# Moving two pair turns, the block table and the totals around expert block 0

## What is computed

```python
# attention: q, k, v [2, 8, 768, 64]; window |i-j| < 16, and 24 block summaries
scores = concat(where(near, q@k.T/8, -1e9), q@k_max.T/8 + log(32))
x = softmax(scores) @ concat(v, v_mean)             # -> x [1536, 512]
# MoE: 8 experts, 512 -> 1024 -> 512
logits = normed(x) @ normed(emb).T / tau
e = argmax(logits); gate = softmax(logits)[e]
x = gate * (relu(x @ w1[e]) @ w2[e])
# dense: 512 -> 2048 -> 512
h = relu(x @ w_in);  out = (h * h) @ w_out
```

## Time and profile before

| | |
|---|---|
| median of 3 runs (lowest, highest) | 553.02 (552.63, 553.21) |
| the profiled execution, its span | 553.05, 551.3 |
| PE busy | 523.8 (95% of the span), 4442 matmuls |
| DVE busy | 269.4 (49%) |
| ACT busy | 234.9 (43%) |
| POOL busy | 89.0 (16%) |
| chain that ended last: PE, SP's queue, DVE, DMA | 84%, 5%, 4%, 4% |

### The profile page before, as it was taken

How to read it: one execution, slowest core, us unless ns; L and a number is a source line. 1 busy time by engine, 2 the same in 40 slices (tenths; PEclk the granted TensorE clock), 3 DMA queues, 4 the chain that set the end, 5 groups by cost and what they waited for, 6 DMA issues and landing times.

```text
span 551.3 us, 10956 instructions
## 1 busy us (share of the span) xinstructions
PE 523.8 (95%) x4442; PEld 473.1 (86%) x4442; DVE 269.4 (49%) x442; ACT 234.9 (43%) x413; POOL 89.0 (16%) x123
## 2 busy tenths in 40 slices
PE   7498977899999999999999999999999999999997
PEld 6387866789998989989889899899989989989995
DVE  6477877768485864757462232232223223232321
ACT  5478855655676653555531231222223123122221
POOL 5761111212543131260100000000000000000000
PEclk9789999899999999999999999999999999999999
DMA  7956678895679958768110020020001002001001
GB/s 215 257 154 176 186 182 251 251 338 176 251 260 331 312 160 275 263 229 275 64 47 1 0 77 1 1 76 0 0 21 56 0 0 76 0 0 38 2 2 38
DMA packets 62655, 69.50 MB, mean 126 GB/s; under 512 B 22512, under 2 KB 47088, under 8 KB 62232
## 3 DMA queue, kind: packets, MB, share of 16 engines
q1 hardware_dynamic: 59160, 57.36, 32.9%
q0 software_dynamic: 3456, 11.60, 6.2%
HBM read 58.88 MB, written 10.06 MB: 125 GB/s over the span
## 4 chain that ended last, share of the span: by engine, by line
PE 84%; SPq 5%; DVE 4%; DMA 4%; issue 1%; ACT 1%; POOL 0%; DVEq 0%; ACTq 0%; POOLq 0%
PE psum L917 26%; PE psum L918 25%; PE psum L919 25%; DMA k_raw<-in_k 2%; SPq L364 2%; PE psum L911 1%; PE psum L765 1%; PE psum L703 1%; DMA x_rows_sb<-x_rows,gather_tab 1%; SPq L366 1%; PE psum L1021 1%; SPq L363 1%; DVE wb_lo L1627 1%; DVE neg_max L1351 1%; PE psum L830 1%
## 5 line engine op out<-in xcount | busy, mean ns | idle before, releaser
L919 PE MATMUL psum<-x_hi,win_lo 128*128 128x256 f32 x384 | 108.7, 283 | 0.0
L918 PE MATMUL psum<-x_lo,win_hi 128*128 128x256 f32 x384 | 108.7, 283 | 0.0
L917 PE MATMUL psum<-x_hi,win_hi 128*128 128x256 f32 x384 | 108.5, 282 | 0.0
L1725 DVE TENSOR_TENSOR h_sq<-h_relu 128x512 f32<-128x512 f32 x48 | 33.2, 692 | 126.6 <-ACT h_relu L1291 126.6
L1291 ACT ACTIVATE h_relu<-psum 128x512 f32<-128x512 f32 x48 | 28.7, 597 | 127.4 <-PE psum L919 127.4
L917 PE MATMUL psum<-wb_hi,h_hi 128*128 128x512 f32 x208 | 82.4, 396 | 0.0
L919 PE MATMUL psum<-wb_hi,h_lo 128*128 128x512 f32 x208 | 81.1, 390 | 0.0
L918 PE MATMUL psum<-wb_lo,h_hi 128*128 128x512 f32 x208 | 81.1, 390 | 0.0
L918 PEld LDWEIGHTS psum<-x_lo,win_hi 128*128 128x128 f32 x384 | 73.6, 192 | 1.4
L917 PEld LDWEIGHTS psum<-x_hi,win_hi 128*128 128x128 f32 x384 | 73.6, 192 | 1.4
L919 PEld LDWEIGHTS psum<-x_hi,win_lo 128*128 128x128 f32 x384 | 73.6, 192 | 0.0
(11 more groups left out here) (211 smaller groups left out, 878.2 us busy)
## 6 DMA issues: line engine op xcount, KB each, us to landing
w_raw<-in_moe_w SPq DMA_DIRECT2D x56, 512.0 KB, 4.0
win_raw<-in_moe_w_in POOLq DMA_DIRECT2D x8, 512.0 KB, 8.1
w_raw<-in_moe_w_out SPq DMA_DIRECT2D x8, 512.0 KB, 3.6
k_raw<-in_k SPq DMA_DIRECT2D x8, 384.0 KB, 3.6
q_raw<-in_q SPq DMA_DIRECT2D x8, 384.0 KB, 5.5
v_blk<-in_v SPq DMA_DIRECT2D x3, 1024.0 KB, 8.0
v_win<-in_v SPq DMA_DIRECT2D x16, 192.0 KB, 3.9
x_rows<-x_all SPq DMA_DIRECT2D x8, 384.0 KB, 5.4
```

Source lines behind the costliest of these rows:

```text
L917: pe.matmul(o, l_hi, r_hi, start=start, stop=False)
L918: pe.matmul(o, l_hi, r_lo, start=False, stop=False)
L919: return pe.matmul(o, l_lo, r_hi, start=False, stop=stop)
L1725: dve.tensor_tensor(h_sq[c % 2][:, :], h_relu[c % 2][:, :], h_relu[c % 2][:, :], ALU.mult)\
```

## The change

Routing of batch 0, in the attention's last pairs:

- `choose` is split: `read_logits` (L1487) stays in place, `row_max(3,0,0)` and `move_prob(2,1,0)` come next, then the rest of `choose(0)`.
- PE's `totals` moves behind `values(2,1,0)` and `turn_pair(4)`, from the free end of bank 5 to bank 7; it waits for DVE's copy of the last q and k out of that bank, and DVE's `move_totals` moves behind `move_pair(4)`. `fill(3,1,2)`, the next writer of bank 7, waits for `totals_moved`; before, `turn_pair(4)` did.
- `lay_blocks` is split: `lay_starts` (L1522 to L1533) stays, and the table of experts moves behind `make_hots` and `scale_out(3,0,0)`. `row_max(3,1,1)` moves behind `list_tokens`.
- `hot_tok` of batch 0 goes from DVE to POOL, ahead of the first gather in POOL's program; PE's `slots` waits for it (`toks_made`).

Turning of pairs 5 and 6: out of the attention, to behind piece 0 of block 0's up product. Pair 7 goes from behind piece 0 to behind piece 1, the logits of batch 1 from piece 1 to 2, their turning from piece 2 to 3 and into bank 5. DVE's `choose(1)` moves behind the whole up product, `totals(1)` from step (0,0) of the down product to (0,3), `ranks(1)` from (0,3) to (1,0). PE's wait for `logits_read` moves from ahead of `turn_rows(1)` to step (0,6).

Loads of block 0: before, four pieces were issued ahead of the store of x of pair 6 and the wait for the first rows; now two are.

```diff
 # SP, load_expert
-                    if first and c == PIECES:
+                    if first and c == PIECES // 2:
                         store_x(PAIRS - 2)
                         sp.wait_ge(gathered, 32)
 # POOL, ahead of gather(0)
+            pool.wait_ge(hot_hi_made, 1)
+            pool.tensor_tensor(hot_tok[:, :, :], hot_hi[:, :, :],
+                               token1[:, 0:TILES].unsqueeze(2).broadcast_to([P, TILES, HB]), ALU.mult)\
+                .then_inc(toks_made, 1)
+            pool.wait_ge(toks_made, 1)
 # PE
+            values(2, 1, 0)
+            turn_pair(4)
             pe.wait_ge(consts_made, 2)
-            pe.wait_ge(prob_moved[0], 2 * 5 + 1)
-            pe.wait_ge(prob_moved[1], 2 * 5 + 1)
-            totals(0, 5, at=GT * P)
-            values(2, 1, 0)
-            pe.wait_ge(totals_moved, 1)
-            turn_pair(4)
+            pe.wait_ge(qk_moved_dve, PAIRS)
+            totals(0, 7)
...
+            pe.wait_ge(totals_moved, 1)
             fill(3, 1, 2)
...
-            turn_pair(5)
             scores(3, 1, 1)
-            wait_turned(6)
             turn_probs(3, 0, 1)
+            pe.wait_ge(toks_made, 1)
             slots(0, 7)
...
-            turn_pair(6)
-            wait_turned(7)
             turn_probs(3, 1, 1)
 # PE, weigh_second
                 if c == 0:
...
+                    turn_pair(PAIRS - 3, bank=6)
+                    turn_pair(PAIRS - 2, bank=4)
+                elif c == 1:
+                    wait_turned(PAIRS - 1)
                     turn_pair(PAIRS - 1, bank=6)
-                elif c == 1:
+                elif c == 2:
                     wait_turned(PAIRS)
                     logits(6)
-                elif c == 2:
-                    turn_logits(1, 7)
+                else:
+                    turn_logits(1, 5)
 # PE, count_second
-                if (t, f) == (0, 0):
+                if (t, f) == (0, 3):
                     totals(1, 0)
-                elif (t, f) == (0, 3):
+                elif (t, f) == (0, FC - 2):
+                    pe.wait_ge(logits_read, 2)
+                elif (t, f) == (1, 0):
                     ranks(1, 1)
 # ACT and DVE, block 0
             for c in range(PIECES):
-                if c == 3:
-                    choose(1, 7)
                 experts_up(0, c)
                 if c == 0:
+                    move_pair(PAIRS - 3, bank=6)
+                    move_pair(PAIRS - 2)
+                elif c == 1:
                     move_pair(PAIRS - 1, bank=6)
-                elif c == 1:
+                elif c == 2:
                     move_logits(1, 6)
+            read_logits(1, 5)
+            choose(1)
```

DVE's program for the last pairs, cut:

```diff
             move_logits(0, 4)
+            read_logits(0, 5)
+            row_max(3, 0, 0)
+            move_prob(2, 1, 0)
             dve.wait_ge(consts_made, 2)
-            choose(0, 5)
-            move_prob(2, 1, 0)
-            row_max(3, 0, 0)
+            choose(0)
             move_kq(3, 1)
-            move_totals(0, 5, at=GT * P)
             scale_out(2, 1, 0)
             move_pair(4)
+            move_totals(0, 7)
...
-            lay_blocks(0, 7)
+            lay_starts(0, 7)
             row_max(3, 1, 0)
             place(0, 7)
             make_hots(0)
             scale_out(3, 0, 0)
+            lay_blocks(0)
+            list_tokens(0, 7)
             row_max(3, 1, 1)
-            list_tokens(0, 7)
             scale_out(3, 0, 1)
```

More of the change, by code:

```diff
@@ L276, in build @@
         hots_made = sem("hots_made")
+        placed = sem("placed")
+        hot_hi_made = sem("hot_hi_made")
+        toks_made = sem("toks_made")
         slots_made = sem("slots_made")
@@ L991, in _ @@
             expert_up(0, first=True, behind=weigh_second)
-            pe.wait_ge(logits_read, 2)
             turn_rows(1)
@@ L1191, in _ @@
             exps(3, 1, 0)
-            move_pair(5)
-            move_pair(5, half=1)
             move_prob(3, 0, 1)
             move_prob(3, 0, 1, hh=1)
+            move_prob(3, 1, 0)
             exps(3, 1, 1)
-            move_prob(3, 1, 0)
-            move_pair(6)
+            move_prob(3, 1, 1)
             def split_hi(dst, made, c, count, loads):
@@ L1253, in _ @@
             split_hi(wa_hi, wa_hi_made, 0, 0, 16)
-            move_prob(3, 1, 1)
             move_x(0, bank=0)
@@ L1481, in move_logits, with read_logits, choose @@
                    .then_inc(logits_moved, 1)
-            def choose(b, bank):
+            def read_logits(b, bank):
                 dve.wait_ge(logits_done, b + 1)
-                mine = margin[:, b * TILES:(b + 1) * TILES, :]
                 dve.tensor_scalar(rt[:, 0, :, :], ps_logit(bank), tau_sb[:, 1:2], None, ALU.mult)\
                    .then_inc(logits_read, 1)
+            def choose(b):
+                mine = margin[:, b * TILES:(b + 1) * TILES, :]
                 dve.wait_ge(logits_read, b + 1)
@@ L1516, in move_totals, with lay_starts @@
                 dve.tensor_copy(tot_t[:, :], ps_tot(bank, at)).then_inc(totals_moved, 1)
-            def lay_blocks(b, bank):
+            def lay_starts(b, bank):
                 of = rb[:, b, :, :]
@@ L1533, in lay_blocks @@
                 link(dve.tensor_tensor(of[:, 3, :], begin, of[:, 0, :], ALU.add))
+            def lay_blocks(b):
+                of = rb[:, b, :, :]
                 link(dve.tensor_tensor(cmp_b[:, :, :], of[0:1, 3, :].unsqueeze(1).broadcast_to([1, MAXB, E]),
@@ L1562, in place @@
                 dve.tensor_copy(rs[:, 6, :], ri[:, 2, :])
-                link(dve.tensor_copy(rs[:, 5, :], ri[:, 1, :]))
+                dve.tensor_copy(rs[:, 5, :], ri[:, 1, :]).then_inc(placed, 1)
+                dve.wait_ge(placed, b + 1)
             def make_hots(b):
@@ L1568, in per_column @@
                     return a.unsqueeze(2).broadcast_to([P, TILES, width])
-                link(dve.tensor_tensor(hot_hi[:, :, :], halves[:, :].unsqueeze(1).broadcast_to([P, TILES, HB]),
-                                       per_column(rs[:, 6, :], HB), ALU.is_equal))
-                dve.tensor_tensor(hot_tok[:, :, :], hot_hi[:, :, :],
-                                  per_column(token1[:, b * TILES:(b + 1) * TILES], HB), ALU.mult)
+                dve.tensor_tensor(hot_hi[:, :, :], halves[:, :].unsqueeze(1).broadcast_to([P, TILES, HB]),
+                                  per_column(rs[:, 6, :], HB), ALU.is_equal).then_inc(hot_hi_made, 1)
+                if b == 1:
+                    dve.wait_ge(hot_hi_made, 2)
+                    dve.tensor_tensor(hot_tok[:, :, :], hot_hi[:, :, :],
+                                      per_column(token1[:, b * TILES:(b + 1) * TILES], HB), ALU.mult)
                 dve.tensor_tensor(hot_lo[:, :, :], lanes[:, :].unsqueeze(1).broadcast_to([P, TILES, P]),
@@ L1691, in _ @@
             for c in range(PIECES):
-                if c == 3:
-                    choose(1, 7)
                 experts_up(0, c)
                 if c == 0:
+                    move_pair(PAIRS - 3, bank=6)
+                    move_pair(PAIRS - 2)
+                elif c == 1:
                     move_pair(PAIRS - 1, bank=6)
-                elif c == 1:
+                elif c == 2:
                     move_logits(1, 6)
+            read_logits(1, 5)
+            choose(1)
             move_x(1)
             move_totals(1, 0)
-            lay_blocks(1, 1)
+            lay_starts(1, 1)
+            lay_blocks(1)
             place(1, 1)
```

## The result

The changed kernel took 557.49 us (median of 4 runs, 556.91 to 558.48) against 553.12 for the kernel before (4 runs, 552.63 to 553.75): ratio 1.007, interval 1.0048 to 1.0092. It is slower. On a second chip, where runs of one kernel lie further apart, it took 556.37 (9 runs, 555.06 to 560.16), ratio 1.0044 (1.0015 to 1.0073). The prediction's 554.0 was too low, and the range, which ended at 556.0, did not hold the time.

The account below looks back on a forecast made before the run. PE was taken as bound from the landing of block 0's first rows, which DVE's routing chain and the gather set. 553.05 - 1.8 (landing) + 2.0 (block 0) + 0.75 (block 1's entry) = 554.0; range 551.5 to 556.0.

Parts of the forecast that it names:

- Part 1: Routing chain on DVE ahead of the gathers: slot copy at 89.3 instead of 91.50, 2.2 earlier.
- rival D: `hot_tok` on POOL starts behind `hot_lo`, takes over 0.9; slots and landing about 0.5 late: 554.5, chance 0.07.
- Part 2: Landing of the second gather: 6.0 from issue, so block 0's rows land at 97.9, 1.8 earlier.
- Part 3: Block 0 on PE: two pair turns (1.14) plus a 0.9 wait for pair copies cost 2.0.
- Rival B: Late loads share the queues with the gather: gather 6.7, block 0 costs 3.1, total 556.0; chance 0.22.
- Rival E: Gather not held up by queued transfers, lands in 5.57 or less, 2.3 earlier: 553.5; chance 0.14.
- Part 4: Entry of block 1: later `ranks` of the second batch make PE wait 0.75 for DVE's first low half.

Follow-up runs that it names:

- e4: The kernel before with two weight pieces instead of four ahead of the first rows, nothing else; 554.29 us, ratio to before 1.0023.
- e10: The kernel before with pairs 5 and 6 turned in block 0 and batch 1's logits, choice, totals and ranks placed as changed; 555.77 us, ratio 1.0050.
- e11: The kernel before with the x store of pair 6 moved behind block 0's eight weight pieces on SP's queue; 551.97 us, ratio 0.9966.
- e9: The changed kernel with pairs 5 and 6 back in the attention and the block table laid directly behind the block starts; 554.24 us, ratio to before 1.0015.
- e5: The changed kernel with batch 1's ranks moved ahead of column group 5 of block 0's first half of tokens; 555.26 us, ratio to before 1.0027.

## Why the prediction was wrong

**Part 1, the routing chain: right in size.** Slot copy 2.2 earlier predicted; against the two traces of before it is 2.7 and 1.7. The forecast took as given that L1496 is stretched to 1.20; of the five traces with the old order only two have that, the other three have 0.21. `hot_tok` on POOL did stretch: 1.23 beside `hot_lo`, against 0.72 for a 128x256 one, and PE's `slots` waited 0.55 for it. That mechanism of rival D is real, but its price is nothing, since DVE came to the slots 0.3 later (slots done at 90.18, copy at 90.47). POOL's op began beside `hot_lo` (88.05 against 87.88) and ended 0.45 behind it. By the rule of the Trainium skill, SBUF — State Buffer, section "SBUF: two separate sides", the one holds the other up. The trace agrees in that POOL needed 1.23 for what 0.72 bounds when it is alone. That the op stood for the whole of `hot_lo`, as I had read the rule, it does not show: the 0.45 behind `hot_lo` is less than the op takes alone. `choose` no longer lies beside the POOL copy: L1508 takes 0.21, has 1.20.

**Part 2, the landing: the step that failed.** "I take 6.0, close to its own row, since its own place already had full queues." The queues were indeed full there: the DMA engines were 0.86 busy between that gather's issue and the turn of its rows, more than the 0.77 of the changed kernel. But I took full queues for a state with one price, and the price is what is still to be moved. In the kernel before SP asked for its four pieces from 87.16 on, seven ahead of the second gather, and most of them were through: 1.26 and 1.12 MB were left to move, the gathers included, and the rows took 5.70 and 5.53. In the changed kernel three transfers are asked for within 1.6 of the gather, 1.89 and 1.90 MB are to be moved, and it takes 7.5 to 7.9 in four traces and 7.06 in a fifth. An estimate from these figures: 0.7 MB more, at the 0.35 MB per us that the engines reach when busy, is 2.0. The rows were turned 27.4 and 27.3 behind the logits turn, where before it was 28.1 and 26.9: by the means 0.15 earlier instead of 1.8. Of the 2.2 won on DVE, 2.0 went back to the queue. The row that should have ended the choice was among those quoted: 7.7 for a gather asked for while pieces were moving. Rival B had the mechanism and priced it 6.7, one too low; its 556.0 came nearest. Rival E said no delay at all: 5.37 and 5.50 with 0.92 MB to move against 7.7 with 1.9 decide against it. The Trainium skill, DMA: Bandwidth & Descriptors, section "Queues, rings and completion order", says only in what order a DMA engine serves its queues, by turns and a packet at a time. That SP's backlog would then not matter was my own conclusion.

**Part 3, block 0: the right chain, sized too short.** PE's wait is there, 0.79 (0.9), and so is the chain that ends it: third weight piece, cast, low half, pair copies. But the turn of pair 7 comes 11.9 behind the landing in the first trace and 12.2 in the second, where I had 11.4. The third piece was there 7.8 behind the landing (7.6) in the first and 8.2 in the second, and from there to the turn of pair 7 it takes 4.1, not 3.8. That is most of what made the sum of 2.0 into 2.6 to 2.9 against before's 18.1. The rest, 0.1, lies behind the wait. By parts: the turns alone 1.7, two pieces alone 1.4, which is e4's wait of 1.42; together they cost less than the sum, because what PE has more to do ahead of the wait shortens it. "PE's half clock does not enter" holds for the changed kernel: with 4.1, 6.0 and 0 at half clock PE waited 0.79, 0.26 and 1.49, and the copies set the end each time. It does not hold where PE has no wait: in e10 PE came 0.5 later to the turn of pair 7 than its own work explains (10.92 instead of 9.85 and 0.57), with 4.2 at half clock instead of 2.9, and e11 lost 1.2 so.

How long the clock stays at half is not set by the wait for the rows alone: 2.9 behind an idle time of 1.97 (before), 5.9 behind 1.70 (e11), 5.7 behind 0.79 (e9), 4.1 behind 6.19 (after).

**Part 4, the entry of block 1: 1.1 against 0.75.** Cause shown by e5. DVE's wait for the ranks grew from 2.49 to 4.36, and because `lay_starts`, `lay_blocks` and `place` lie between the ranks and block 1's first low half, all of it was passed on.

**The sum again.** -1.8 became -0.15, 2.0 became 2.7, 0.75 became 1.1: 3.65 instead of 0.95, by the mean of two traces each. With 553.05 this is 556.7, between the two measured medians' 557.5 and 555.4 (553.0 times 1.0044). The error of 2.7 is the landing's 1.65, block 0's 0.7 and the entry's 0.35.

## What to carry to other kernels

When a step is moved, look at which transfers it releases and what they will then run beside: making the index list early and the weight table late exchanged 2.2 us on VectorE for 2.0 us on the queue. Price such a transfer by the bytes that are still to be moved when it is issued, and not by whether the queues are full. A transfer on which the next stage waits wants an empty path, so ask first whether something unimportant stands next to it (here the store of a pair whose rows are first gathered at 151, 58 us later); moving that one line won 0.34%, where the reordering lost 0.4 to 0.7%. And work moved from an engine's gaps into its dense part costs its duration plus every wait that it brings: two pair turns of 1.14 together cost 2.8. When an experiment meets the number of a theory, look whether the waits moved as the theory says: the run that kept TensorE busy met its number while PE's wait had grown.

## What the runs showed of the hardware

- The second of two indirect gathers of 128 rows took longer the more the DMA engines had to move from its issue on, the gathers' own 0.52 MB included: 0.9 to 1.0 MB, 4.45 to 6.40 from issue to use (six traces); 1.1 to 1.3 MB, 5.5 to 5.7 (three); 1.4 and 1.5 MB, 6.4 and 6.3; 1.7 MB, 7.20; 1.9 MB, 7.06 to 7.91 (five). The same arrangement gave 5.37 and 6.40 in two traces, so a single trace prices it badly.
- With TensorE idle for 6.2 and 6.1 the granted clock fell to 0.50 ahead of the work and stayed there for its first 4.1 and 6.0 us. In the kernel before, behind 1.97 and 1.89, it was at half for 2.9 and 3.4. Where PE had no wait behind the rows, 3.0 more at half clock cost it 1.2 (e11 against before).
- A 128x240 tensor_tensor on POOL took 1.23 beside a two-input one on DVE, and a 128x256 one 0.72 alone. A small two-input DVE operation (128x48) took 1.20 and 1.16 beside a POOL copy, 0.21 otherwise.
- The same instructions reach the same point 5.2 us apart in different executions (69.7 to 75.0 at the logits turn). One trace can't price a change of 0.5%; stretches behind a common point agreed within 0.3 over most of them.
